# Pooling the first batch's q and k out of the turned PSUM banks, with the order of loads, of kept output blocks and of two later turns that goes with it

## The reference, cut to what matters

```python
# attention: q, k, v are [4 batches, 8 heads, 576 tokens, 64]
q_d = q.reshape(B, H, 144, 4, 64).mean(axis=3)      # k_d and v_d alike: four tokens pooled into one
out_up = repeat(sm_attn(q_d, k_d, v_d), 4)          # pooled attention, repeated over the four tokens
out_local = softmax(scores where |i - j| < 4) @ v   # local attention, a band of seven keys
x = (out_up + out_local) as [2304 tokens, 512]
# first gated layer, then a second one
x = ((x @ w_a) * (x @ w_b)) @ w_out                 # 512 -> 1536 -> 512
out = layernorm-like(x @ w_in) @ w_out2             # 512 -> 1024 -> 512
```

## Time and profile before

| | us |
|---|---|
| median of three runs | 809.77 (807.83 to 813.96) |
| the profiled execution's own time | 813.36 |
| its span, first to last instruction | 811.6 |
| busy in the span: PE, DVE, ACT, POOL | 768.3, 559.7, 299.9, 214.3 |

### The profile page before, as it was taken

One profiled execution on the slowest core, in us unless ns is written; L12 is line 12 of the kernel. 1 busy time (PEld: TensorE's weight loads), 2 busy tenths in 40 slices (PEclk: granted clock), 3 DMA queues, 4 the chain that ended last, 5 costly groups with the idle time before them and its releaser, 6 DMA issues.

```text
span 811.6 us, 12276 instructions
## 1 busy us (share of the span) xinstructions
PE 768.3 (95%) x4440; PEld 702.2 (87%) x4440; DVE 559.7 (69%) x969; ACT 299.9 (37%) x819; POOL 214.3 (26%) x258
## 2 busy tenths in 40 slices
PE   6987789899979999998999999999999999999998
PEld 5776689799869999997999999999988888888886
DVE  2688699979858787877688687112457666666663
ACT  3542555445242534253353525223522222222212
POOL 3466786518055403014001121121200000000000
PEclk9999999999989999998999999999999999999999
DMA  9999968565847777675465553357110110111111
GB/s 184 217 220 256 245 173 230 156 219 164 248 145 232 253 213 187 170 207 132 116 209 176 176 166 107 120 180 222 64 65 27 53 53 26 53 53 36 43 40 40
DMA packets 94685, 119.14 MB, mean 147 GB/s; under 512 B 17057, under 2 KB 56739, under 8 KB 94625
## 3 DMA queue, kind: packets, MB, share of 16 engines
q1 hardware_dynamic: 79904, 108.85, 48.2%
q10 hardware_dynamic: 14721, 9.51, 4.1%
HBM read 97.49 MB, written 20.84 MB: 146 GB/s over the span
## 4 chain that ended last, share of the span: by engine, by line
PE 73%; POOL 3%; DMA 2%; DVE 0%; issue 0%; ACT 0%; SPq 0%; DVEq 0%; ACTq 0%
PE psum L847 23%; PE psum L849 22%; PE psum L848 22%; PE psum L961 2%; POOL raw L1676 2%; DMA wo_raw<-in_moe_w_out 1%; POOL raw L1680 1%; PE psum L803 1%; DMA raw<-in_q 1%; PE psum L783 1%; PE psum L814 1%; PE psum L793 1%; PE psum L769 0%; POOL wo_lo L1696 0%; DVE tmp L1403 0%
## 5 line engine op out<-in xcount | busy, mean ns | idle before, releaser
L847 PE MATMUL psum<-x_hi,w_hi 128*128 128x384 f32 x576 | 201.7, 350 | 2.5 <-DVE x_lo L1364 2.4
L849 PE MATMUL psum<-x_hi,w_lo 128*128 128x384 f32 x576 | 196.2, 341 | 0.0
L848 PE MATMUL psum<-x_lo,w_hi 128*128 128x384 f32 x576 | 195.9, 340 | 0.0
L847 PEld LDWEIGHTS psum<-x_hi,w_hi 128*128 128x128 f32 x576 | 110.7, 192 | 6.6 <-issue 4.9
L1370 DVE TENSOR_TENSOR ab_f<-psum,a_sb 128x384 f32<-128x384 f32 x72 | 39.8, 553 | 105.8 <-PE psum L849 62.8
L848 PEld LDWEIGHTS psum<-x_lo,w_hi 128*128 128x128 f32 x576 | 111.0, 193 | 0.0
L849 PEld LDWEIGHTS psum<-x_hi,w_lo 128*128 128x128 f32 x576 | 110.6, 192 | 0.0
L847 PE MATMUL psum<-ab_hi,wo_hi 128*128 128x384 f32 x288 | 100.9, 350 | 3.0 <-issue 2.9
L849 PE MATMUL psum<-ab_hi,wo_lo 128*128 128x384 f32 x288 | 97.1, 337 | 0.0
L848 PE MATMUL psum<-ab_lo,wo_hi 128*128 128x384 f32 x288 | 97.0, 337 | 0.0
L1676 POOL TENSOR_TENSOR raw<-raw 96x256 f32<-96x256 f32 x60 | 59.4, 1015 | 103.2 <-DMA raw<-in_q 51.9
(11 more groups left out here) (143 smaller groups left out, 1417.4 us busy)
## 6 DMA issues: line engine op xcount, KB each, us to landing
wo_hi<-wo_hi_scratch SPq DMA_DIRECT2D x54, 256.0 KB, 2.7
wo_lo<-wo_lo_scratch SPq DMA_DIRECT2D x54, 256.0 KB, 3.1
k_u<-in_k SPq DMA_DIRECT2D x11, 576.0 KB
v_u<-in_v SPq DMA_DIRECT2D x11, 576.0 KB
k_u<-in_k SPq DMA_DIRECT2D x17, 288.0 KB
v_u<-in_v SPq DMA_DIRECT2D x17, 288.0 KB
raw<-in_v SPq DMA_DIRECT2D x8, 576.0 KB, 8.5
raw<-in_q SPq DMA_DIRECT2D x8, 576.0 KB, 11.6
```

What stands on the lines that cost most here:

```text
L847: mm(dst, wh, xh, start=first, stop=False, skip_group_check=not check)
L848: mm(dst, wh, xl, start=False, stop=False, skip_group_check=not check)
L849: last = mm(dst, wl, xh, start=False, stop=end, skip_group_check=not check)
```

## The change

- **Head.** q and k of batch 0 are loaded once, all 576 tokens, as 256-byte pieces (`q_h` and `k_h` have six blocks of 96 rows). PE turns six blocks each, q into banks 0 and 1, k into banks 6 and 7. `qT` and `kT` are copied out in two pieces. DVE adds groups of four columns straight from the banks (`head_sums`, two reductions a pair), and scales the pooled q once (`head_scale`). The raw tiles of q and k of batch 0, `head_pool`, and batch 0's `turn_qk` and `qk_copy` are gone. The next `head_turn` waits for these sums.
- **Order.** Pooled scores, maxima and exponentials of pairs 0 and 1 stand between the local parts of pairs 1 to 3. `head_up(0)` and `head_up(1)` now come before the pooled scores of pairs 2 and 3, and `head_up(0)` stands ahead of `head_values(3)`.
- **SP.** `load_wo(0)` goes ahead of `store_vd(0, ...)`; `q_u` and `k_u` go right behind it; `load_wo(1)` and `load_weights(1)` come before raw v of batch 1; `load_wo(2)` and raw q of batch 1 come behind that.
- **w_out.** Tile 0 keeps blocks 7 to 11; tile 1 loads blocks 0 to 6 fresh and keeps them.
- **Later slots.** In tile 1 the turns of batch 2's q move from slot 25 to 28. In tile 3 the turns of batch 3 move one slot on, two pooled jobs (12 to 13, 17 to 18) and two loads (`xup`, `v_u`) with them.

```diff
-        (3, 0, "R", 2, 0), (3, 5, "R", 2, 2), (3, 12, "R", 3, 0), (3, 17, "R", 3, 2),
+        (3, 0, "R", 2, 0), (3, 5, "R", 2, 2), (3, 13, "R", 3, 0), (3, 18, "R", 3, 2),
...
-QK_AT = {0: {10: (4, 5), 11: (6, 7)}, 1: {25: (8, 9)}, 2: {0: (10, 11)}, 3: {10: (12, 13), 11: (14, 15)}}
+QK_AT = {0: {10: (4, 5), 11: (6, 7)}, 1: {28: (8, 9)}, 2: {0: (10, 11)}, 3: {11: (12, 13), 12: (14, 15)}}
...
+FIRST_KEPT = 7
 def wo_fresh(g):
     m, j = divmod(g, FC)
-    return m == 0 or (m == 1 and j % 2 == 1)
+    return m == 0 or (m == 1 and j < FIRST_KEPT)
 def wo_kept(g):
     m, j = divmod(g, FC)
-    return wo_fresh(g) and m == j % 2
+    return wo_fresh(g) and (m == 0) == (j >= FIRST_KEPT)
...
-    raw_head = raw + [place(f"raw{2 + i}", [PPB * BLK, 2, 3, R4 * D], FP32, o)
-                      for i, o in enumerate((k_at, tmp_at, v_at, acc_at))]
+    raw_head = [place(f"raw{2 + i}", [PPB * BLK, 2, 3, R4 * D], FP32, o) for i, o in enumerate((v_at, acc_at))]
...
-    q_h = place("q_h", [IQ, 4, DM], FP32, o)
-    k_h = place("k_h", [IK, 5, DM], FP32, o + 8192)
-    qT = place("qT", [128, 2, NT], FP32, o + 18432)
-    kT = place("kT", [128, 2, PAD + KN + 1], FP32, o + 24576)
-    band = place("band", [2 * QR, 2, WIN], FP32, o + 27808)
-    loc_min = place("loc_min", [2 * QR, 2, LT], FP32, o + 28384)
-    loc_sum = place("loc_sum", [2 * QR, 2, LT], FP32, o + 28448)
-    loc_den = place("loc_den", [2 * QR, 2, LT], FP32, o + 28512)
-    loc_inv = place("loc_inv", [2 * QR, 2, LT], FP32, o + 28576)
+    q_h = place("q_h", [IQ, 6, DM], FP32, o)
+    k_h = place("k_h", [IQ, 6, DM], FP32, o + 12288)
+    qT = place("qT", [128, 2, NT], FP32, o + 24576)
+    kT = place("kT", [128, 2, PAD + KN + 1], FP32, o + 27648)
...
-    RAW_PASS = [(0, 0), (1, 2), (1, 1), (2, 2), (2, 0), (2, 1), (3, 2), (3, 1)]
+    RAW_PASS = [(1, 2), (1, 1), (2, 2), (2, 0), (2, 1), (3, 2), (3, 1)]
...
-                                 q[0, c + 4 * hh, 0:NT, :].rearrange("(t p) d -> p t d", p=IQ)
+                                 q[0, c + 4 * hh, :, :].rearrange("(t p) d -> p t d", p=IQ)
...
-                                 k[0, c + 4 * hh, 0:KN, :].rearrange("(t p) d -> p t d", p=IK)
+                                 k[0, c + 4 * hh, :, :].rearrange("(t p) d -> p t d", p=IQ)
...
-            for tau in (2, 0, 1):
-                load_raw(0, tau, 0)
-                load_raw(0, tau, 1)
+            load_raw(0, 2, 0)
+            load_raw(0, 2, 1)
             load_weights(0)
+            load_wo(0)
             store_vd(0, 0)
             store_vd(0, 1)
-            load_wo(0)
+            load_unit_q(1, 0)
+            load_unit_k(1, 0)
             load_vd(0)
+            load_wo(1)
+            load_weights(1)
             load_raw(1, 2, 0)
             load_raw(1, 2, 1)
-            sp.wait_ge(s.qk_turned, 4)
-            load_unit_q(1, 0)
-            load_unit_k(1, 0)
-            load_wo(1)
+            load_wo(2)
             load_raw(1, 0, 0)
             load_raw(1, 0, 1)
-            load_weights(1)
-            load_wo(2)
             store_vd(1, 0)
             store_vd(1, 1)
...
-                            if n == (18 if rest else 13):
+                            if n == (18, 13, 13, 19, 13)[m]:
                                 load_xup(m + 1, 0)
-                            if n == (19 if rest else 14):
+                            if n == (19, 14, 14, 20, 14)[m]:
...
-                wait_qT(c - 1)
+                at_least(pe, s.qd_summed, c)
                 pe.wait_ge(q_h_loaded[c], 32)
-                for t in range(4):
-                    last = turn(bank(0)[:, t * IQ:(t + 1) * IQ], q_h[:, t, c * 128:(c + 1) * 128], ident[0:IQ, 0:IQ])
+                for t in range(6):
+                    last = turn(bank(t // 3)[:, t % 3 * IQ:(t % 3 + 1) * IQ], q_h[:, t, c * 128:(c + 1) * 128],
+                                ident[0:IQ, 0:IQ])
                 last.then_inc(s.h_turned, 1)
...
+                at_least(pe, s.kd_ready, c)
                 pe.wait_ge(k_h_loaded[c], 32)
-                for t in range(5):
-                    last = turn(bank(1)[:, t * IK:(t + 1) * IK], k_h[:, t, c * 128:(c + 1) * 128], ident[0:IK, 0:IK])
+                for t in range(6):
+                    last = turn(bank(6 + t // 3)[:, t % 3 * IQ:(t % 3 + 1) * IQ], k_h[:, t, c * 128:(c + 1) * 128],
+                                ident[0:IQ, 0:IQ])
...
-                    pe.wait_ge(s.qk_out, 4)
-                if c == 1:
-                    wait_qT(PPB - 1)
-                    pe.wait_ge(s.kT_ready, PPB)
+                    pe.wait_ge(s.kd_ready, PPB)
+                    pe.wait_ge(s.qd_ready, 1)
...
-            turn_qk(0, 6)
+            head_pooled_scores(0)
+            head_pooled_scores(1)
             head_turn_p(2)
-            turn_qk(1, 7)
             head_values(2)
-            turn_qk(2, 6)
+            head_turn_pooled(0)
             head_turn_p(3)
-            turn_qk(3, 7)
-            head_values(3)
-            for c in range(PPB):
-                head_pooled_scores(c)
-            head_turn_pooled(0)
             head_turn_pooled(1)
             head_up(0)
+            head_values(3)
+            head_up(1)
+            head_pooled_scores(2)
+            head_pooled_scores(3)
...
-                A(qT[:, c % 2, :], bank(0, NT), ACT.Copy).then_inc(s.qT_by_scalar, 1)
+                A(qT[:, c % 2, 0:3 * IQ], bank(0, 3 * IQ), ACT.Copy)
+                A(qT[:, c % 2, 3 * IQ:], bank(1, NT - 3 * IQ), ACT.Copy).then_inc(s.qT_by_scalar, 1)
...
-            qk_copy(0, 6)
             head_exp(3)
             head_pT(2)
-            qk_copy(1, 7)
-            qk_copy(2, 6)
-            head_pT(3)
-            qk_copy(3, 7)
             head_pooled_exp(0)
             head_pooled_exp(1)
-            head_pooled_exp(2)
+            head_pT(3)
             head_pooled_pT(0)
-            head_pooled_exp(3)
             head_pooled_pT(1)
             weight_high(0)
+            head_pooled_exp(2)
+            head_pooled_exp(3)
+            x_high(0, 0)
+            x_high(0, 1)
...
+            def sum_rows(dst, banks, c):
+                src = psum[:, banks * BANK:(banks + 2) * BANK].rearrange("p (b n) -> p b n", b=2)[:, :, 0:3 * IQ]
+                return V.tensor_reduce(dst[:, c * SD:(c + 1) * SD].rearrange("p (b n) -> p b n", b=2),
+                                       src.rearrange("p b (n r) -> p b n r", r=R4), AX.X, ALU.add)
+            def head_qT(c):
+                dve.wait_ge(s.h_turned, 2 * c + 1)
+                V.tensor_copy(qT[:, c, 0:3 * IQ], bank(0, 3 * IQ))
+                V.tensor_copy(qT[:, c, 3 * IQ:], bank(1, NT - 3 * IQ)).then_inc(s.qT_by_vector, 1)
             def head_kT(c):
                 dve.wait_ge(s.h_turned, 2 * c + 2)
                 at_least(dve, s.h_scored, c - 1)
-                V.tensor_copy(kT[:, c % 2, PAD:PAD + KN], bank(1, KN)).then_inc(s.kT_ready, 1)
+                V.tensor_copy(kT[:, c % 2, PAD:PAD + 3 * IQ], bank(6, 3 * IQ))
+                V.tensor_copy(kT[:, c % 2, PAD + 3 * IQ:PAD + KN], bank(7, KN - 3 * IQ)).then_inc(s.kT_ready, 1)
+            def head_sums(c):
+                sum_rows(kdT, 6, c).then_inc(s.kd_ready, 1)
+                if c > 0:
+                    dve.wait_ge(s.qT_by_scalar, c)
+                sum_rows(qdT, 0, c).then_inc(s.qd_summed, 1)
+            def head_scale():
+                dve.wait_ge(s.qd_summed, PPB)
+                V.tensor_scalar(qdT[:, :], qdT[:, :], POOLED_SCALE, None, ALU.mult).then_inc(s.qd_ready, 1)
...
-            V.tensor_copy(qT[:, 0, :], bank(0, NT)).then_inc(s.qT_by_vector, 1)
+            head_qT(0)
             head_kT(0)
+            head_sums(0)
             dve.wait_ge(s.band_ready, 1)
             head_mask(0)
             head_kT(1)
+            head_sums(1)
             head_mask(1)
             head_inverse(0)
             head_kT(2)
+            head_sums(2)
             head_inverse(1)
             head_mask(2)
             head_local(0)
             head_kT(3)
-            head_pool(0, 0)
+            head_sums(3)
+            head_scale()
             head_inverse(2)
             head_mask(3)
             head_local(1)
-            head_pool(0, 1)
+            head_pooled_max(0)
+            head_pooled_max(1)
             head_inverse(3)
-            head_pool(1, 0)
             head_local(2)
-            head_pool(1, 1)
+            head_pooled_norm(0)
+            head_pooled_norm(1)
+            weight_low(0, WA)
             head_local(3)
-            for c in range(3):
-                head_pooled_max(c)
-            head_pooled_norm(0)
+            head_pooled_max(2)
             head_pooled_max(3)
-            for c in range(1, PPB):
-                head_pooled_norm(c)
-            weight_low(0, WA)
             for c in range(2):
                 head_x(c)
+            head_pooled_norm(2)
+            head_pooled_norm(3)
```

More of the change, by code:

```diff
@@ L47 @@
 WIN = QR + 2 * PAD
-IQ, IK = 96, 80
-KN = 5 * IK
+IQ = 96
+KN = 400
 HEAD_BLOCKS = 2
```

(43 more changed lines are left out.)

17 lines of the change are left out of this document (9 added, 8 removed).

## The result

The kernel after takes **800.07 us** (median of 4 executions, 797.57 to 801.89) against 808.98 in the same series: a ratio of 0.9878, 95% interval 0.9833 to 0.9922. That is faster by 1.2%; the forecast of 789.3 was 10.8 us too low, inside its range of 780 to 801 by 0.9 us. The profiled execution took 798.9 us (span 797.1) against 813.36 before.

The account below looks back on a forecast made before the run. Memory was taken to bound at most the head and tile 0; tiles 1 and 3 carried waits. Head and tile 0 -7.0, tile 1 -9.2, tile 3 -4.3 sum to -20.5 us: 813.4 to 792.9, as median 789.3; range 780 to 801.

Parts of the forecast that it names:

- Tile 1: PE's waits for x and POOL's raw q and the lower clock go, less 1 us of new costs: -9.2 us.
- (c): Tile 1's wait moves to tile 2's first slot, for late raw k of batch 2: 795 us, chance 0.08.
- (e): ACT stands for a fresh w_out block in each of five tile 1 blocks: slower, 830 us, chance 0.05.
- Tile 3: Turns one slot later shorten PE's wait for POOL and avoid the lower clock, less 0.7 us: -4.3 us.
- The head: v_d arrives later, at about 43.5, so the first product starts near 53 instead of 48.5 us.
- (d): Small pieces move at half the rate, 118 GB/s, so v_d and w_lo come 10 us later: 799, chance 0.04.
- +1.7: From the head into tile 0: raw q of batch 1 lands 1 to 2 us later, costing 1.7 us.
- -8.7: Further in tile 0: ACT's two w_out waits go (-5.1), a lower clock (-1.2) and two further waits (-2.4).
- an end of +8: Upper end of the +1.7 step: v's store takes 12 us and holds back everything behind load_vd.
- (b): Tile 0 gives back the full 15 us of bytes: 781 us, chance 0.10.
- (a): DVE and POOL, not DMA, pace tile 0, so head delay and gains cancel there: 796 us, chance 0.18.
- 3.6 us: Step from profiled time to median: the profiled execution lay this much above the runs' median, turning 792.9 into 789.3.

Follow-up runs that it names:

- second edit: Kernel before with only the new rule for which w_out blocks are kept: 804.93 us, ratio 0.9924 to before.
- eighth experiment: Kernel after with SP's load of v_d ahead of q_u and k_u: 800.73 us, ratio 0.9884 to before.
- (6): Kernel after with POOL adding only a third of the rows of batch 1's raw tiles: 793.38 us, ratio 0.979 to before.
- (10): Kernel after with v and q of batch 1 both loaded and pooled earlier, whole computation kept: 792.54 us, ratio 0.9777 to before.
- (9): Kernel after with v of batch 1 loaded ahead of the stores of the pooled v and pooled at once: 796.13 us, ratio 0.9828 to before.
- (7): Kernel after with POOL's low parts of block 2 ahead of its passes over q of batch 1: 801.17 us, ratio 0.9881 to before.
- 12: Kernel before with POOL adding only a third of the rows of batch 1's raw tiles: 808.97 us, ratio 0.9972 to before.
- (5): Kernel after with tile 0's local scores for tile 1's tokens over 32 of 64 dimensions on DVE: 797.76 us, ratio 0.9837 to before.
- 11: Kernel after with both tile 0's local scores over 32 of 64 dimensions and a third of POOL's batch 1 rows: 794.04 us, ratio 0.9791 to before.

## Why the prediction was partly right

**Tile 1: right.** Forecast -9.2, profiled -8.5. No L769 wait is left there. The two edits share it: the slots alone give 4.2 us of tile 1, the rule alone 7.9, both 8.3. The price I put at 1 us for fresh blocks in a row shows as ACT waits of 0.86, 1.64 and 3.37 us for w_out, with no PE wait over 1.2 us behind them. Rivals (c), a wait at tile 2's first slot, and (e), ACT standing long in every block, fell.

**Tile 3: right in kind, a little small.** Forecast -4.3, profiled -5.9: no part of the wait stayed, where I had left 1.4 us. The size of this term can't be told better from single profiles: with the old slots tile 3 took 93.2, 93.1, 89.8 and 89.1 us in four kernels, with the new ones 87.3 to 89.1. Where it took 93, the granted clock was 0.58 (before) and 0.56 (second edit) in the 6.9 us behind the wait of 3.5 and 3.4 us, for the most part the lower level of 1.2 GHz; where it took 89 to 90 with the old slots, that wait was 1.4 us and the clock stayed at 1.00.

**The head: the direction right, the size off.** First product at 55.98, not 53. v of batch 0 was pooled at 33.0 (I said near 34) and v_d was issued at 38.77 (I said 39.5), but it came at 46.6, not 43.5, behind `q_u` and `k_u`. The DMA share from 30 to 40 us was 0.44: the idle time was there, 5.6 us of it. By the eighth experiment little of this counted for the end: with the first product 6.3 us earlier, tile 0 ended 0.7 us earlier.

Rival (d) named 799, the figure nearest to the measured one, and is wrong all the same: from 5 to 10 and from 10 to 15 us, before the first raw tile is issued at 15.39, the kernel after moved 193 and 204 GB/s in small pieces, not 118. The prediction's own stretch for them in the kernel before, 10 to 15 us, was not as pure as it said, since SP issued raw v at 12.15 there; the rate holds. So does its reading of the earlier trace rows, but for the last twelve slices, which read 26 to 65 GB/s and not 27 to 64.

**Tile 0: the step that failed**, the +1.7 and the -8.7 with it. The mechanism of the -8.7 was real: ACT's waits for w_out fell from 6.58 and 4.21 us to none and 1.41, and PE's waits for `p_pool` and `pT_pool` went. Of the 7.5 us by which the first product is late, 3.4 came back before ACT's first copy `a_sb` (56.05 in before, 60.20 in after). From there to the fifth copy before took 44.8 us (to 100.88) and after 41.1 (to 101.27): 3.8 us came back, and the rest of the later start took them. The +1.7 was sized by the bytes up to raw q of batch 1 ("it lands 1 to 2 us later"). But what is late at `w_lo` of block 2 is POOL's sum, and that begins with raw v. The diff moves v's load behind `q_u`, `k_u` and a pair of weight blocks: it is issued at 42.43 for 37.90, and POOL begins at 55.06 for 44.41. Before, 9.4 us of pooling lay in front of the landing of q; after, q was there first, and `w_lo` came at 75.62, 8.4 us later for the 1.7 I took. I had named an end of +8 for another cause, a slow store. The fault is that a load moved in SP's queue was priced by its bytes, not by the work on POOL that starts with it.

That POOL's passes behind the moved load hold tile 0 of after is shown: less work for POOL (6), and the same work earlier (10), bring the end of tile 0 forward by 6.6 and 5.6 us, with times clear of after's interval, and (9), half of that move, by 3.5 us; a different order at the same place (7) doesn't. How much of it runs through `w_lo` and how much through SP, whose weights for block 4 wait behind the same passes (65.99, against 59.30 and 57.68 in 6 and 10), these runs don't separate. Rival (b), all bytes won back, fell. Rival (a) said that DVE and POOL pace tile 0. For before it is wrong about POOL (12: less POOL work gives nothing while the queue is full), and DVE wasn't tried there. For after it is right about POOL. For DVE it was tested twice (5, 11) and gave 2.6 us at the most.

**The rest of the miss** is the step from profiled time to median. I took off 3.6 us because before's profiled execution lay that much over its median. After's lay 1.2 us under its own, and in later series before's median was 810.6 to 811.6. Of the 10.8 us, 6.0 are in the terms (-14.5 for -20.5), and 4.8 in that difference of two single executions. That the time still fell inside the range is luck as far as tile 0 goes: the upper end was drawn for (a) and (d), and tile 3 gave 1.6 us more than forecast.

**Open:** why fewer stores (2) gave tile 0 nothing although it waited for transfers. From 46 to 98 us the DMA share was 1.06 to 1.10 (1.05 to 1.10 in before), while 214 to 236 GB/s were moved instead of 219 to 259, so the queue was no emptier; what it spent the time on wasn't tried. And in every kernel block 4 to the first copy of tile 1 takes 60 to 64 us: 62.2 in after, 60.5 with less POOL work (6), 60.2 with less DVE work (5). PE in before and after is busy for 13.1 to 13.7 of each 14 us from 112 to 154 us there, and DVE for 13.0 to 13.9. What sets this stretch is not settled.

## What to carry to other kernels

When a stage has several limits within a few microseconds of each other (here transfers, POOL and DVE), price a change by the second limit, not by the first: what is taken from the queue is worth only what the next engine can use. For each load that a diff moves, follow the engine whose work starts with it and ask whether its time was hidden in a wait that the move removes. An engine's long idle stretch just before it becomes late is the place to move its work to: two pairs of loads issued earlier gave 7.5 us here, about as much as the later slots alone (1.0%) and more than the new rule for w_out (0.8%).
